# Low parts of the left-over tokens placed in the empty rows of the token mix's fifth tile, with the first load and the last stores cut in halves

## What is computed

```python
scores = scale * q @ k.T + bias           # per head, key 0 to 127 positions back
x = softmax(scores) @ v                   # heads side by side: x is (4, 576, 512)
h = x.transpose(0, 2, 1) @ U @ V          # U is (576, 32), V is (32, 576)
u = x + h.transpose(0, 2, 1)              # the token mix
x2 = u + relu(u @ w_ch1) @ w_ch2
out = (gated MLP of x2)                   # w_in, w_spatial, b_spatial, w_out
```

## Time and profile before

| what | value |
|---|---|
| median of 3 runs | 717.57 us (716.21, 717.57, 717.58) |
| the profiled execution's own time | 718.08 us |
| its span, first to last instruction | 716.3 us |
| mean granted TensorE clock | 0.998 |
| TensorE matmuls busy | 705.1 us, 98% |
| VectorE busy | 452.4 us, 63% |
| ScalarE busy | 339.0 us, 47% |
| GpSimd busy | 178.9 us, 25% |

### The profile page before, as it was taken

How to read it: one execution, slowest core, us unless ns; L and a number is a source line. 1 busy time by engine, 2 the same in 40 slices (tenths; PEclk the granted TensorE clock), 3 DMA queues, 4 the chain that set the end, 5 groups by cost and what they waited for, 6 DMA issues and landing times.

```text
span 716.3 us, 12975 instructions
## 1 busy us (share of the span) xinstructions
PE 705.1 (98%) x4624; PEld 659.8 (92%) x4624; DVE 452.4 (63%) x1032; ACT 339.0 (47%) x765; POOL 178.9 (25%) x183
## 2 busy tenths in 40 slices
PE   8999999999999999999999999999999999999998
PEld 5677777789999999999999999999898998998997
DVE  6979797898673274339868967976384354354341
ACT  5888788864352243234443444444352432432422
POOL 2498646510009807650050000000010100100100
PEclk9999999999999999999999999999999999999999
DMA  7659974055547856799276175468800100100101
GB/s 215 194 194 395 366 277 143 17 191 177 220 147 266 303 181 217 263 384 382 92 244 217 45 264 183 156 216 283 336 1 1 67 0 0 66 0 0 66 1 67
DMA packets 72145, 122.46 MB, mean 171 GB/s; under 512 B 4896, under 2 KB 43808, under 8 KB 71584
## 3 DMA queue, kind: packets, MB, share of 16 engines
q1 hardware_dynamic: 72096, 121.82, 49.1%
HBM read 74.29 MB, written 47.51 MB: 170 GB/s over the span
## 4 chain that ended last, share of the span: by engine, by line
PE 75%; DVE 4%; ACT 0%; issue 0%; DVEq 0%
PE bank L1917 8%; PE bank L1919 8%; PE bank L1918 8%; PE bank L1959 4%; PE bank L1961 4%; PE bank L1960 4%; PE wide L1959 3%; PE wide L1961 3%; PE wide L1960 3%; PE bank L2068 2%; PE bank L2070 2%; PE bank L2069 2%; PE bank L1884 2%; PE bank L1882 2%; PE bank L1883 2%; PE wide L1883 2%
## 5 line engine op out<-in xcount | busy, mean ns | idle before, releaser
L1917 PE MATMUL bank<-xs,w1s 128*128 128x384 f32 x336 | 113.0, 336 | 1.0 <-DVE tok L1442 0.8
L1919 PE MATMUL bank<-xs,w1s 128*128 128x384 f32 x336 | 112.3, 334 | 0.0
L1918 PE MATMUL bank<-xs,w1s 128*128 128x384 f32 x336 | 112.3, 334 | 0.0
L1075 ACT ACTIVATE rk<-tok 128x768 fp32r<-128x768 f32 x72 | 61.0, 849 | 71.3 <-PE bank L1961 32.4
L916 POOL TENSOR_TENSOR vl<-vr,vh 128x512 fp32r<-128x512 f32 x8 | 11.3, 1407 | 291.9 <-ACT vh L1200 291.9
L1053 ACT ACTIVATE sums_u<-bank 128x384 f32<-128x384 f32 x72 | 35.4, 491 | 88.7 <-PE bank L1919 88.5
L929 ACT ACTIVATE sc<-sc,mn 128x256 f32<-128x256 f32 (+1 forms) x144 | 67.0, 469 | 18.6 <-DVE mn L1260 18.4
L1959 PE MATMUL bank<-rk,w2q 128*128 128x384 f32 x208 | 69.9, 336 | 0.3 <-DVE rk L1464 0.3
L1960 PE MATMUL bank<-rk,w2q 128*128 128x384 f32 x208 | 69.5, 334 | 0.0
L1961 PE MATMUL bank<-rk,w2q 128*128 128x384 f32 x208 | 69.5, 334 | 0.0
L1917 PEld LDWEIGHTS bank<-xs,w1s 128*128 128x128 f32 x336 | 63.1, 188 | 2.7 <-issue 1.3
(11 more groups left out here) (212 smaller groups left out, 1822.1 us busy)
## 6 DMA issues: line engine op xcount, KB each, us to landing
r_scr<-tok SPq DMA_DIRECT2D x20, 768.0 KB, 3.9
tok<-r_scr SPq DMA_DIRECT2D x15, 768.0 KB, 7.1
w1raw<-w SPq DMA_DIRECT2D x32, 256.0 KB, 3.9
w2q<-w_scr SPq DMA_DIRECT2D x4, 2048.0 KB, 11.1
wc_scr<-wprep SPq DMA_DIRECT2D x12, 512.0 KB, 6.5
w_scr<-tok SPq DMA_DIRECT2D x11, 512.0 KB, 3.8
qkraw<-qk SPq DMA_DIRECT2D x16, 320.0 KB, 5.0
qkraw<-qk SPq DMA_DIRECT2D x16, 288.0 KB, 3.8
```

Source lines behind the costliest of these rows:

```text
L1075: act.activation(rk[:, n % RING, 0], raw(g, RAW_OF[m])[:, 2 * j:2 * j + 2, :], ACT.Relu if m <= 3 else ACT.Copy).then_inc(rk_hi, 1)
L1917: pe.matmul(o, wh, ah, start=(k == 0 and m in FRESH), stop=False, skip_group_check=True)
L1918: pe.matmul(o, wl, ah, start=False, stop=False, skip_group_check=True)
L1919: last = pe.matmul(o, wh, al, start=False, stop=(k == 1), skip_group_check=True)
```

## The change

- `mix_down` drops the product of the fifth tile with `xl`. In its place the fifth tile's rows 64 to 127 of `xh` hold the low part of its tokens, and the same rows of `ust` hold the same rows of U as 0 to 63 (U's last 64 rows are loaded twice, `mix_in` counts 112 in place of 96, and the clearing of `uraw` goes). One matmul then sums the high and the low part.
- `lo_x` on GpSimd computes only four tiles. A new `lo_tail` on VectorE writes the low part of the 64 left-over tokens: 64 partitions by 128, from `xn` and `xh`, both in SBUF. It waits for `x_hi` and stands between `add_u` and `sums` of the step; those of pairs 14 and 15 stand in the hand-written list behind the loop. `mix_down` also waits for it (`x_tail`).
- The first pair's operands come in four DMAs; the first two (128 KB each) are what `scores_x` of pair 0 needs, on a semaphore of their own.
- The last batch's results are stored in eight DMAs of 144 KB in place of four of 288 KB.
- Three semaphores are merged with others.

```diff
-        xl = sb(pa, "xl", [P, TILES, DM], F32R)
+        xl = sb(pa, "xl", [P, TILES - 1, DM], F32R)
+        pa.enter_context(nc.sbuf_tensor("gap1", [P, DM], F32))
...
-            load_qk(0, 0)
+            for c in (slice(0, KEYS), slice(S, S + KEYS)):
+                sp.dma_start(qkraw[:, 0, c], qk[0, 0, :, c]).then_inc(qk_first, 16)
+            for c in (slice(KEYS, S), slice(S + KEYS, 2 * S + TAIL)):
+                sp.dma_start(qkraw[:, 0, c], qk[0, 0, :, c]).then_inc(qk_in[0], 16)
             load_qk(0, 1)
...
-            sp.dma_start(uraw[0:TAIL, TILES - 1, :], mu[full:S]).then_inc(mix_in, 16)
+            for r in (0, TAIL):
+                sp.dma_start(uraw[r:r + TAIL, TILES - 1, :], mu[full:S]).then_inc(mix_in, 16)
...
-            for b in range(B):
+            for b in range(B - 1):
                 store(b)
-            sp.wait_ge(stored, 16 * KD * B)
+            for n in range(2 * KD):
+                t, here = n % 2 * HALF, (B - 1) * S + n % 2 * HALF
+                sp.wait_ge(o_kept, (B - 1) * 2 * KD + n + 1)
+                sp.dma_start(out_t[BATCH[B - 1], n // 2 * P:(n // 2 + 1) * P, t:t + HALF],
+                             tok[:, n // 2, here:here + HALF]).then_inc(stored, 16)
+            sp.wait_ge(stored, 16 * KD * (B + 1))
...
-                pool.tensor_tensor(xl[:, :, c], xn[:, i % 2], xh[:, :, c], ALU.subtract).then_inc(x_split, 1)
+                full = TILES - 1
+                pool.tensor_tensor(xl[:, :, c], xn[:, i % 2, 0:full], xh[:, 0:full, c],
+                                   ALU.subtract).then_inc(x_split, 1)
...
-            pool.memset(uraw[TAIL:P, TILES - 1, :], 0.0).then_inc(tail_set, 1)
-            pool.wait_ge(tail_set, 1)
...
+            def lo_tail(b, i):
+
+                p, c, full = b * PAIRS + i, slice(i * P, (i + 1) * P), TILES - 1
+                dve.wait_ge(x_hi, p + 1)
+                dve.tensor_tensor(xh[TAIL:P, full, c], xn[0:TAIL, i % 2, full, :], xh[0:TAIL, full, c],
+                                  ALU.subtract).then_inc(x_tail, 1)
...
                     add_u(b - ago, k, pt_ps)
+                if two:
+                    lo_tail(*back(b, i, 2))
                 if one:
                     sums(*back(b, i, 1))
...
             lo_first(5)
+            lo_tail(B - 1, 2)
             normalise(B - 1, 3)
...
             lo_first(4)
+            lo_tail(B - 1, 3)
             c11(0)
...
-                pe.wait_ge(qk_in[s], 32 * (b * 2 + i // 2 + 1))
-                if not (isinstance(b, int) and p == 0):
+                if isinstance(b, int) and p == 0:
+                    pe.wait_ge(qk_first, 32)
+                else:
+                    pe.wait_ge(qk_in[s], 32 * (b * 2 + i // 2 + 1))
                     pe.wait_ge(scored, p * NT)
...
                 pe.wait_ge(x_split, (b + 1) * PAIRS)
+                pe.wait_ge(x_tail, (b + 1) * PAIRS)
                 pe.wait_ge(tok_kept, (b + 1) * PAIRS)
-                for t in range(TILES):
+                for t in range(TILES - 1):
                     u = ust[:, t].rearrange("p a r -> p (a r)")
                     pe.matmul(t_ps[:, :], u, xh[:, t, :], start=(t == 0), stop=False)
-                    last = pe.matmul(t_ps[:, :], u, xl[:, t, :], start=False, stop=(t == TILES - 1))
-                last.then_inc(t_done, 1)
+                    pe.matmul(t_ps[:, :], u, xl[:, t, :], start=False, stop=False)
+
+                pe.matmul(t_ps[:, :], ust[:, TILES - 1].rearrange("p a r -> p (a r)"), xh[:, TILES - 1, :],
+                          start=False, stop=True).then_inc(t_done, 1)
```

More of the change, by code:

```diff
@@ L243, in sem @@
             return ctx.enter_context(nc.semaphore(name))
+        qk_first = sem("qk_first")
         qk_in = [sem(f"qk_in{i}") for i in range(2)]
@@ L260, in program @@
         bsp_in = sem("bsp_in")
-        tail_set = sem("tail_set")
         pads_set = sem("pads_set")
@@ L269, in program @@
         dve_passed = sem("dve_passed")
-        mvar_set = sem("mvar_set")
         mix_hi = sem("mix_hi")
@@ L288, in program @@
         x_split = sem("x_split")
+        x_tail = sem("x_tail")
         t_done = sem("t_done")
@@ L868, in _ @@
             pool.wait_ge(dist_done, 3)
-            pool.memset(uraw[TAIL:P, TILES - 1, :], 0.0).then_inc(tail_set, 1)
-            pool.wait_ge(tail_set, 1)
-            pool.memset(vraw[TAIL:P, :, TILES - 1, :], 0.0).then_inc(tail_set, 1)
-            pool.wait_ge(tail_set, 2)
+            pool.memset(vraw[TAIL:P, :, TILES - 1, :], 0.0).then_inc(pads_set, 1)
+            pool.wait_ge(pads_set, 2)
             pool.wait_ge(mix_hi, 1)
@@ L969, in hi_mix @@
             def hi_mix():
-                act.wait_ge(mix_in, 96)
-                act.wait_ge(tail_set, 1)
+                act.wait_ge(mix_in, 112)
                 for r in (0, 2, 3):
@@ L1700, in gates @@
                         lo_g(b, n - 1)
-            dve.memset(mvar[:, :, :], 1.0).then_inc(mvar_set, 1)
-            dve.wait_ge(mvar_set, 1)
+            dve.memset(mvar[:, :, :], 1.0).then_inc(blank_set, 1)
+            dve.wait_ge(blank_set, 2)
             norm_v(0)
@@ L1730, in scores_z @@
                 s = i % 2
+                if isinstance(b, int) and b * PAIRS + i == 0:
+                    pe.wait_ge(qk_in[s], 32)
                 pe.matmul(z_ps[:, 0:TAILKEYS], qkraw[:, s, S + (TILES - 1) * P:2 * S + TAIL],
@@ L1767, in values @@
                 if isinstance(b, int) and p == 0:
-                    pe.wait_ge(tail_set, 2)
+                    pe.wait_ge(pads_set, 2)
                 pe.wait_ge(pt_third, p + 1)
```

## The result

| | before | after |
|---|---|---|
| median on one chip, 8 runs each | 717.33 us (716.21 to 717.8) | 719.63 us (718.69 to 720.72) |
| ratio after / before, 95% | 1 | 1.0036 (1.0026 to 1.0045) |
| profiled execution, its span | 718.08, 716.3 us | 720.13, 718.3 us |

The changed kernel is 0.36% slower: 2.3 us by the medians beside each other, 2.0 us by the two spans. The forecast was 719.9.

The account below looks back on a forecast made before the run. The prediction took TensorE, its matmuls busy 98% of the span, as the bound. Its terms, 0.2 + 3.1 - 0.96 = +2.3 us, added to the median of 717.57 gave 719.9 us; range over all cases 716.0 to 721.4.

Parts of the forecast that it names:

- The rival of VectorE slipping past: GpSimd yields to `lo_tail`, whose cost hides in VectorE's waits; only gains are left, 716.1 us; chance 0.20.
- The half-blocked rival: `lo_tail` waits for GpSimd's operation in progress, but `den` follows it at once: 717.4 us; chance 0.23.
- The third rival: GpSimd's subtraction goes ahead of `lo_tail`, so `mix_down` comes 1.4 us later in place of 0.3: 721.0 us; chance 0.12.
- The first load's -0.49: At the start, halved loads land before the warm-up products end, removing TensorE's whole wait of 0.49 us.
- Pairs 0 and 2, +1.0: `lo_tail` meets GpSimd and delays TensorE by 0.6 us at pair 0 and 0.4 at pair 2.
- Pairs 4 and 8, 1.1 and 1.3: `lo_tail` waits for GpSimd's subtraction, `den` for its CAST; TensorE loses 1.1 us at pair 4, 1.3 at pair 8.
- Pairs 5 and 6, 0.2 each: `lo_tail` meets the CAST's last moments, only `den` meets the subtraction; between 0 and 0.45 us each, 0.2 taken.
- Pair 7 and `mix_down`: `mix_down` waits for pair 7's `lo_tail`, 0.3 us taken; with the matmul saved, 0.07 us predicted for the stretch.
- Pairs 9 to 13 at nothing: GpSimd has no more work of that moment behind `lo_x`, so `lo_tail`'s 0.20 us hides in VectorE's 0.30 us wait.
- The matmul's 0.23 us: One matmul less in a `mix_down` on a packed TensorE gains 0.23 us; batches 1 and 2 together 0.46.
- Pairs 14 and 15 at nothing: In the tail, GpSimd has no more work of that moment behind `lo_x`, so `lo_tail` costs nothing there.
- The last stores, -0.50: At the end, last stores in halves gain 0.50 us, with ends 0 and 0.58.

Follow-up runs that it names:

- the kernel with fills: The changed kernel with GpSimd's CAST and subtraction of `split_wc` replaced by zero fills: 716.61 us, ratio 0.999; the same edit in the kernel before: 716.5 us.
- the edges alone: The kernel before with only the first load and the last stores in halves, nothing of the mix: 717.22 us beside 717.94, ratio 0.9989.

## Why the prediction was right, and where it was not

*The mechanism* was right: a VectorE operation with two SBUF inputs, put where GpSimd is at work, costs over 1 us in place of 0.28 at pairs 2, 4, 8 and 15, and the next small operation often a second wait, though it has one SBUF input only. The rival of VectorE slipping past fell at pair 4 (1.18 us), pair 8 (1.35) and in the kernel with fills, where the loss went with GpSimd's reads. The half-blocked rival fell at pairs 5 and 6, where `den` waited 1.21 us. The third rival did not come: at pair 7 `lo_tail` (83.59) went ahead of GpSimd's subtraction (83.93). Of the signs that were named, the waits of TensorE behind pairs 4 and 8 came out at 0.25 and 0.55 us and not at 1, and the first score products started at 4.91 and not at 4.7.

*The first load's -0.49* failed as a step. The wait existed in the profile and was read as the kernel's. With the same load whole four other executions had no wait, and in three of them, as in the kernel after, the products behind were drawn out to 1.5 us or more. The products at 8.12 in the kernel after stand 0.43 us later than those of before (7.69); it is ahead only because the latter took 2.08 us at the lower clock. So the table's -0.51 beside the predicted -0.49 is luck. A part of a gain there can go into the next wait for a load: it was 0.27 us at 52.62 and is 0.44 after, and 0.76 with the edges alone.

*Pairs 0 and 2, +1.0:* measured about nothing. At pair 0, `den` had already been waiting 0.85 us at 23.60 before the change, which I had not looked at; after it `lo_tail` took 0.58 and `den` 0.59, and one of the four bias operations behind it was spared its turn (0.28 us in place of 0.84), with GpSimd 0.28 us earlier:

```profile
23.20 0.58 DVE L1316 TENSOR_TENSOR xh<-xn,xh 64x128 fp32r<-64x128 f32 x1
23.81 0.59 DVE L1285 TENSOR_SCALAR den<-sm 128x9 f32<-128x9 f32 x1
...
27.69 0.63 PE L1783 MATMUL bank<-ident,sc 128*128 128x128 f32 x4 [1.27 <-DVE pt L1278]
```

*Pairs 4 and 8, 1.1 and 1.3:* measured 0.64 and 0.74. `lo_tail`'s block was sized about right (1.18 and 1.35 us), `den`'s was not: at pair 4 it took 0.47 us, 0.3 more than alone, where 0.6 was added. That makes 1.5 us more on VectorE at pair 4 against 1.9 predicted, and 1.7 at pair 8 against 2.1 by the same working. These 0.4 us each are most of what was missing; the rest is slack that I had read too small.

*Pairs 5 and 6, 0.2 each:* measured 0.45 and 0.46. Here I had set the row of 146.41 against the order of issue and was wrong. The last `lo_x` was held out only while VectorE's subtractions followed one another without a gap: in the timeline they overlap by up to 0.08 us (149.46 starts before 149.13 + 0.41), whereas `lo_tail` and `den` start 0.03 or 0.04 us behind their predecessor's end, and there GpSimd gets in. That this gap decides is inferred from such rows and wasn't tested by itself.

The Trainium skill ("SBUF — State Buffer", Who interferes with whom) says that the shared ports are an exclusive lock and that the order of issue decides who blocks. The trace agrees at pairs 5 and 6 (1.21 us each); its upper figure of 0.45 each was the right one. It doesn't at 148.32, where `lo_x` was released and yet held out by subtractions of VectorE that began later. The same section says that an operation of VectorE with at most one SBUF input, outside the 2-port perf modes, doesn't contend, and that one with two contends only with a GpSimd instruction that reads. Both held for `lo_tail`: 0.28 us with an input from PSUM beside `lo_x`, and 0.28 us beside fills. `den` reads one SBUF input and waited all the same, beside subtractions (1.21 us) and beside fills (0.61 us); no row says in which mode it ran.

*Pair 7 and `mix_down`:* 0.07 predicted, 0.15 measured; TensorE waited 0.27 us before `mix_down` at 84.10, 0.10 us behind `lo_tail`'s end.

*Pairs 9 to 13 at nothing:* right for `lo_tail` itself (0.28 or 0.29 us each), not for what stands behind it. The matmul's 0.23 us doesn't show as a gain there: the offset is 1.79 behind pair 8, 1.93 at pair 11 and 1.92 behind it:

```profile
118.26 0.28 DVE L1316 TENSOR_TENSOR xh<-xn,xh 64x128 fp32r<-64x128 f32 x1
118.37 1.89 POOL L738 TENSOR_TENSOR tok<-tok 128x768 f32<-128x768 f32 x1 [0.88 <-DVE tok L1325]
118.58 1.71 DVE L1285 TENSOR_SCALAR den<-sm 128x9 f32<-128x9 f32 x1
118.65 0.47 PE L1840 MATMUL wide<-xh,ust 128*128 128x512 f32 x1 [0.19 <-issue]
```

GpSimd's sum of 1.89 us, released by VectorE's own `add_u`, was pending when `lo_tail` ended and went ahead of `den`, which before had passed in 0.16 us. I had called these pairs free because `split_wc` is over by then, and had not looked for GpSimd's sums. That this wait ate the matmul's gain is argued from the rows and wasn't tested by itself.

*Pairs 14 and 15 at nothing:* the step that missed most. I priced them by the rule "no `split_wc` behind them" and didn't look at `lo_x` itself, which the earlier trace rows show running late, over the very place where `lo_tail` stands. It cost 1.0 us in the profile; the kernel with that one line moved had it back.

*The last stores, -0.50:* measured 0.7 us, ten profiles against four.

The Trainium skill ("DMA: Bandwidth & Descriptors", Anatomy of one DMA) gave 0.34 us by its 2.0 us and 436 GB/s. That section is on DMAs issued by GpSimd, and these stores are issued by SyncE, which the prediction left out. The stores of 144 KB landed in 1.7 us and those of 288 KB in 2.1, so the slope is 0.4 us for 144 KB and the constant part, an estimate from these two, 1.3 us.

The errors nearly cancelled. Pairs 0, 2, 4 and 8 were priced 1.9 us too dear in all, and the tail, pairs 5 to 7 and pairs 9 to 12 1.9 us too cheap. That the 719.9 came so near the 719.63 is for that reason luck; what the mechanism earned is the sign and the rough size.

## What to carry to other kernels

Before an operation with two SBUF inputs is put on VectorE, list everything GpSimd runs at each of its places, its own last and latest instructions too; if GpSimd already does the neighbouring work and has time, the operation belongs there (here 0.45 us each and 2.8 us less in all, against 2.3 us more with it on VectorE). If it must be on VectorE, one input from PSUM, or a neighbour that only writes, kept this one at 0.28 us. Don't take the small operations behind it for safe: `den`, with one SBUF input, was held up to 1.71 us, and 0.6 us by a mere fill. And a wait of half a microsecond at the start of a profile should be looked for in a second execution before it is counted as a gain.

## What the runs showed that was not expected

A single line's place in the tail (pair 15's `lo_tail` before or after three other operations) decides over 1 us of 718. The start of one and the same code differs by over 1 us between executions: with the load whole the first sums stood at 15.18 and at 16.67 us, with the granted clock at 1.00 throughout in the first and down to 0.50 in the second; why the eight products at 4.91 took 1.53 to 1.66 us in seven profiles and 1.02 to 1.13 in five, at a granted clock of 1.00 in both, stays unexplained. And GpSimd's subtraction of 128x512, 1.28 us elsewhere, was held for 2 us by VectorE operations that ran one right behind the other, while in every row shown here a single one with a gap ahead of it lost its turn to the GpSimd operation that was pending.
